# Special store rows dealt out again over the DMA engines: two more engines take three each, seven take one fewer, one takes one more

## The reference

```python
kv = einsum('bhsd,bhse->bhde', k, v)            # 8 batches, 8 heads, 576 rows, 64 columns
out = einsum('bhsd,bhde->bhse', q, kv)
x = out / rms(out) * g_norm                     # as 4608 tokens x 512
logits = x @ phi                                # 32 slots: 8 experts x 4
slot_input = softmax(logits, over tokens).T @ x
slot_out[e] = relu(slot_input[e] @ w1[e]) @ w2[e]
return softmax(logits, over slots) @ slot_out   # 4608 x 512, float32
```

## Time and profile before

| | |
|---|---|
| median of 3 runs | 171.88 us (171.63 to 171.92) |
| the profiled execution's own time | 171.93 us |
| its span, first to last instruction | 170.6 us |
| outside the span | 1.3 us |
| busy share of the span: PE, ACT, DVE, POOL | 87%, 52%, 51%, 35% |
| DMA engines, mean busy share in nearly all slices | 0.9 or more |
| moved | 71.63 MB, mean 420 GB/s |

### The profile page before, as it was taken

The page is one execution under the profiler, slowest core; times in us unless marked ns, Lnnn a source line. Parts: engine busy times, 40 slices in busy tenths (PEclk is TensorE's granted clock), DMA queues, the critical chain, the costliest instruction groups (busy, mean ns, idle before and its releaser), DMA issues.

```text
span 170.6 us, 3976 instructions
## 1 busy us (share of the span) xinstructions
PE 148.2 (87%) x1704; PEld 100.6 (59%) x1704; DVE 87.4 (51%) x187; ACT 88.8 (52%) x230; POOL 59.4 (35%) x73
## 2 busy tenths in 40 slices
PE   7989699899899899999988999899969889989200
PEld 3469578799679787887885673333326543445000
DVE  1122159583677464857266998526886036318300
ACT  3036587787956888869498870204131045218300
POOL 7000707777456476382736589000000004000000
PEclk9999999999999999999999999999999999999755
DMA  5999999999999999999999899999899999999996
GB/s 184 419 421 424 440 421 438 471 423 444 458 412 423 432 441 447 454 399 454 442 423 454 380 473 414 423 408 460 366 423 434 446 434 401 424 418 422 439 447 259
DMA packets 3843, 71.63 MB, mean 420 GB/s; under 512 B 778, under 2 KB 778, under 8 KB 913
## 3 DMA queue, kind: packets, MB, share of 16 engines
q1 hardware_dynamic: 3425, 71.20, 97.7%
q0 software_dynamic: 400, 0.18, 0.4%
HBM read 61.94 MB, written 9.44 MB: 418 GB/s over the span
## 4 chain that ended last, share of the span: by engine, by line
PE 49%; DMA 29%; ACT 11%; DVE 3%; SPq 2%; issue 1%
PE psum L93 49%; DMA arena<-in_w_dram 15%; DMA arena<-in_kv_dram 14%; ACT arena L93 3%; ACT bd L93 3%; ACT sq L93 2%; SPq L93 2%; ACT part L93 1%; DVE ms L93 1%; ACT r L93 1%; ACT d L93 1%; DVE logits L93 1%; DVE d L93 0%; DVE part L93 0%; DVE arena L93 0%
## 5 line engine op out<-in xcount | busy, mean ns | idle before, releaser
L93 PE MATMUL psum<-bd,arena 128*128 128x192 f32 (+1 forms) x320 | 54.8, 335 | 2.8 <-ACT bd L93 1.6
L93 PEld LDWEIGHTS psum<-bd,arena 128*128 128x128 f32 (+1 forms) x320 | 45.2, 179 | 8.4 <-ACT bd L93 2.8
L93 PE MATMUL psum<-arena 128*64 128x64 f32 (+2 forms) x896 | 36.3, 270 | 1.9 <-DMA arena<-in_kv_dram 1.0
L93 PEld LDWEIGHTS psum<-arena 128*64 128x64 f32 (+2 forms) x896 | 27.5, 129 | 14.6 <-issue 4.8
L93 DVE TENSOR_REDUCE ms<-sq 128x16 f32<-128x1024 f32 (+1 forms) x19 | 22.1, 1163 | 26.5 <-ACT sq L93 26.0
L93 POOL TENSOR_TENSOR arena<-arena,r 128x512 f32<-128x512 f32 x34 | 34.7, 1042 | 0.0
L93 POOL TENSOR_TENSOR part<-part,r 128x512 f32<-128x512 f32 x17 | 17.8, 1048 | 47.9 <-DVE r L93 47.9
L93 ACT COPY arena<-psum 128x512 f32<-128x512 f32 (+2 forms) x48 | 30.7, 649 | 6.0 <-PE psum L93 5.9
L93 ACT ACTIVATE sq<-psum 128x512 f32<-128x512 f32 x36 | 21.5, 597 | 9.6 <-PE psum L93 9.2
L93 ACT COPY part<-psum 128x256 f32<-128x256 f32 (+1 forms) x38 | 13.6, 359 | 12.6 <-DVE part L93 11.4
L93 DVE TENSOR_REDUCE logits<-part 128x64 f32<-128x512 f32 (+1 forms) x18 | 17.8, 991 | 0.1
(11 more groups left out here) (77 smaller groups left out, 110.0 us busy)
## 6 DMA issues: line engine op xcount, KB each, us to landing
arena<-in_w_dram SPq DMA_DIRECT2D x2, 8064.0 KB, 30.2
arena<-in_t_dram SPq DMA_DIRECT2D x1, 6912.0 KB, 37.5
arena<-in_w_dram SPq DMA_DIRECT2D x1, 6400.0 KB, 23.0
arena<-in_w_dram SPq DMA_DIRECT2D x3, 2048.0 KB, 19.2
arena<-in_kv_dram SPq DMA_DIRECT2D x2, 2304.0 KB, 23.7
arena<-in_kv_dram SPq DMA_DIRECT2D x1, 4608.0 KB, 42.8
arena<-in_w_dram SPq DMA_DIRECT2D x1, 4096.0 KB, 25.8
arena<-in_kv_dram SPq DMA_DIRECT2D x1, 3584.0 KB, 32.4
```

The source lines that it names most:

```text
L93: self.inst, self.token = method(*args, **kwargs), None
```

## The change

Special chunk-rows on each engine:

| engine | 0 | 1 to 4, each | 5, 6 | 7, 8, each | 9, 10 | 11, 12, each | 13, 14 | 15 |
|---|---|---|---|---|---|---|---|---|
| before | 11 | 6 | 0 | 10 | 0 | 0 | 0 | 9 |
| after | 10 | 5 | 0 | 9 | 0 | 3 | 0 | 10 |

In all seven chunk-rows are taken, one from each of seven engines, and seven are given: three each to engines 11 and 12, one to 15. The total stays 64. GpSimd's queue issues three stores in place of two: behind the one for 7 and 8 a step of two (over 9 and 10), the store for 11 and 12, another step of two (over 13 and 14), and the store for 15, which now has 5 partitions of both chunks. A step no longer waits for the one before it and reads and writes rows of its own; SP waits for every step at the end. No bytes are added except those of the steps.

```diff
 FIRST = (
-    ("sync", 1, 4, 30, 5, 1, 0, 1), ("sync", 121, 4, 2, 3, 3, 0, 1), ("sync", 117, 4, 3, 2, 2, 1, 2),
-    ("gpsimd", 1, 4, 20, 2, 1, 1, 2), ("gpsimd", 81, 4, 9, 2, 2, 1, 2),
+    ("sync", 1, 4, 25, 5, 1, 0, 1), ("sync", 101, 4, 2, 3, 3, 0, 1), ("sync", 97, 4, 3, 2, 2, 1, 2),
+    ("gpsimd", 1, 4, 18, 2, 1, 1, 2), ("gpsimd", 73, 4, 6, 2, 1, 1, 2), ("gpsimd", 109, 4, 5, 2, 2, 0, 2),
     ("sync", 3, 4, 32, 1, 1, 0, 2), ("sync", 0, 2, 64, 1, 1, 0, 3), ("sync", 1, 2, 64, 1, 1, 2, 3),
 )
-STEPS = (7, 6)
+STEPS = (7, 2, 2)
...
-    stepped_over = [None]
+    stepped_over = []
 
     def step_over(n):
-        ends = [x[:n, : 2 * w].rearrange("p (c n) -> p c n", c=2)[:, :, :4] for x, w in ((stepped, 8), (first_in, 64))]
-        stepped_over[0] = dma(pool, *ends, after=[stepped_over[0]])
+        at = sum(STEPS[: len(stepped_over)])
+        rows = slice(at, at + n)
+        ends = [x[rows, : 2 * w].rearrange("p (c n) -> p c n", c=2)[:, :, :4] for x, w in ((stepped, 8), (first_in, 64))]
+        stepped_over.append(dma(pool, *ends) if n else None)
...
-    for token in [*stores[:-1], stepped_over[0]]:
+    for token in filter(None, [*stores[:-1], *stepped_over]):
         nc.sync.wait_ge(*token)
```

## The result

Over 20 runs each, the changed kernel has a median of 172.23 us against 171.80; the ratio is 1.0018, with a 95% interval of 1.0010 to 1.0025. By the medians it is slower by 0.43 us, a quarter of a per cent; the ratio, which takes all runs with their two levels, is just under a fifth of a per cent. Both are clearly more than nothing.

What follows compares the result with a forecast made beforehand. The prediction took the slowest of 16 DMA engines to bound the kernel. Its terms, 0 + 0.42 + 0 + 0.03, gave +0.45 us on the profiled 171.93, and 172.3 against the median; range 171.8 to 172.65.

Steps and rivals of the forecast that it cites:

- Term 2: Three chunk-rows more on engines 11 and 12 delay the end by +0.42 us, bounds 0 and +0.69.
- lone late start: Profile sign: one or two last packets start alone at 169.6 to 170.0, 0.3 to 0.7 us behind the rest.
- A: The forecast: engine 11 or 12 is among the nine late engines, end moves +0.2 to +0.75 us; chance 0.70.
- C: Engines 11 and 12 have one fetch each and absorb their rows; end unchanged, 171.9 us with small packets; chance 0.12.
- Term 1: One chunk-row fewer on engines 0 to 4, 7 and 8: value 0, bounds -0.23 and 0 us.
- Term 3: One chunk-row more on engine 15: bounds 0 and +0.23 us, nothing in the sum.
- rival B: 11 and 12 are early; engine 15's tenth chunk-row sets the end, +0.1 to +0.23 us; chance 0.13.
- Terms 4, 5 and 6: GpSimd's two more DMA instructions and small packets, +0.03 us; later rows holding up last store, nothing; SP's extra waits, nothing.
- term 4: GpSimd's queue issues two more DMA instructions: later issue costs nothing, added small packets 0 to +0.1 us, taken as +0.03.

Runs made afterwards that it cites:

- six rows: Six chunk-rows on each of engines 11 and 12, three fewer each on 7 and 8, against the changed kernel; 172.76 to 173.20 and two lower, ratio 1.0052.
- the last kernel above: Against the kernel before: one chunk-row fewer on each of eight fetching engines, four more each on 7 and 8, one more on 0, one fewer on 15; 172.61 us.
- 13 and 14 again: Second measurement of the changed kernel with its six chunk-rows on engines 13 and 14 instead of 11 and 12; ratio 1.0027, one run at 171.64.
- 9 and 12: The changed kernel with its six chunk-rows on engines 9 and 12, three each, measured twice; median of all 172.39 us, ratios 1.0030 and 1.0033.
- seven on 12: Seven chunk-rows on engine 12, none on 11, one fewer on engine 0, against the changed kernel; ratio 1.0048, heaps at 171.87 to 172.02 and 172.93 to 173.41.
- one row each, cut astray: One chunk-row each on 11 and 12, taken from 7 and 8, against the kernel before, the two rows one contiguous piece; 173.41 us, ratio 1.0068.
- one row each, mended: One chunk-row each on 11 and 12, taken from 7 and 8, cut so they cannot merge, against the kernel before; 171.91 us, ratio 1.0007.

## Why the prediction was right

**The bound.** That the end is the slowest of 16 DMA engines, and that only the dealing of rows matters, holds in each kernel: moves of a few packets made levels of up to 2 us, and the traces show the last engines alone.

**Term 2, three rows on 11 and 12: +0.42 with bounds 0 and 0.69.** The upper level stands 0.45 above before, and six rows raise it to a median of 173.1, 1.3 above. The step and its size were right for four executions in five. The lone late start that the prediction described, at 169.6 to 170.0, is not in the changed kernel's trace, whose last start is before 169.1; it is in that of the same load on 13 and 14, at 169.6 to 169.7.

**The strings of packets.** In the trace of before, of the 1823 packets that start after 100 us and end before 168, 1814 have another that starts 3 to 5 ns before their end, and at 13 moments from 144 to 166 us 16 packets are under way each time. So the records can be strung into 16 strings, each the work of one engine; where two continuations fit, I take the one with which every string has the even transfers of SP's queue in the same order, eight packets of each. In the trace of before one string then carries 11 special chunk-rows of SP's queue, four carry six, GpSimd's nine for engine 15 are on one, and of its 20 for 7 and 8 ten are on one string, eight and two on two others (a wrong link), as the kernel deals them. With the fetches of a trace numbered 1 to 13 in time, a fetch and the eighth after it are on one string in 58 of 65 cases, in the 13 traces that could be strung so (all but that of the last kernel above), and 6, 7 and 8 have no second one in 38 of 39. That is a turn around eight engines, five of them with two. That they are PE's fetches is inferred from counts: between one and the next PE and its weight loads start 211 to 328 instructions, while ACT, DVE and POOL start 235, 197 and 81 in the whole trace. In the trace of before the strings of 6, 7 and 8 start their last packet at 167.55, 167.75 and 168.05, those of 1 and 9, 4 and 12, 2 and 10 at 168.85, 169.08 and 169.32, and those that carry 11 and 13 at 168.88 and 168.98. In the traces with rows on engines that fetch:

| kernel, traced run | rows: fetches of their strings, last start | last start of all others |
|---|---|---|
| changed, 171.68 | three: 7, 168.09; three: 8, 168.17 | 169.06 (2 and 10) |
| 13 and 14 again, 171.64 | three: 6, 168.75; three: 7, 168.39 | 169.04 (11) |
| 13 and 14, 172.29 | three: 6, 168.29; three: 5 and 13, 169.62 | 169.11 |
| 9 and 12, 172.11 | three: 8, 168.00; three: 3 and 11, 169.51 | 168.91 |
| 9 and 12 again, 172.48 | three: 3 and 11, 169.87; three: none found, 168.17 | 169.11 |
| six rows, 173.17 | six: 3 and 11, 170.56; six: 4 and 12, 170.42 | 169.10 |
| seven on 12, 173.35 | seven: 4 and 12, 170.70 | 169.11 |
| one row each, cut astray, 172.13 | nine: 6, 169.53 | 169.02 |
| one row each, mended, 171.96 | one: 1 and 9, 169.34; one: 2 and 10, 169.29 | 169.17 |

Three rows on a string with one fetch end before the last of the others; three or more on one with two fetches, and nine on one with one, end behind all strings without such rows.

**Rivals A and C.** I set them against each other as one being true. Both are, by the levels: A in 16 of 20 executions, C in 4. The last sentence of the prediction named as a sign of its being wrong that the engines that fetch might change from one execution to the next, and they do. So the picture of one fixed turn was wrong. The median hit all the same because a median shows only the commoner level; had the lower level been the commoner one, the same mechanism would have given some 171.6. The changing turn should have been a rival with a forecast of its own, two levels. The chance of 0.11 that 11 and 12 are both single was too low by the prediction's own picture: the three single engines are neighbours in the turn, which makes it 2 in 8. I read from one trace that 6, 9, 10, 11 and 12 carried two fetches, which came from the packets strung together; strung the same way, the traced run of the changed kernel begins its turn at 13, those of the others at 6, 9, 10 or 11, always in the order of the numbers. In the lower runs whose traces there are (changed kernel, 13 and 14), the loaded pair has one fetch each. In the upper ones that could be strung, at least one has two; with seven rows on 12 the string that carries them has the fetches at 46.9 and 139.0 us and starts its last packet at 170.70, where the next to last string does so at 169.11. No view numbers the engines, and the strings have some wrong links, so this rests on counts and levels as well: low runs 7 of 44 for a neighbouring pair with three or six rows (changed kernel, 13 and 14, six rows), 0 of 11 for the pair that is never single, 9 of 23 for one engine. Equally likely beginnings would give 11, 0 and 8.6. That they are equally likely is not shown: 7 is on the low side of 11 (seven or fewer of 44 would come up with a chance of 0.11).

**Term 1, relief worth nothing, bounds -0.23 and 0.** In the median nothing: the kernel with the rows on 7 and 8 keeps the relief of 0 to 4 and is level with before. The lower level, 0.17 under before's median, may be this relief; four runs are too few to say so.

**Term 3 and rival B, engine 15.** Ten rows there cost nothing (the rows-on-7-and-8 kernel, interval up to 1.0003). By the strings, engine 15 starts its last packet at 169.23 in the trace of before, last but one of all; 7 and 8, with a row more each, do so at 168.07 and 168.28. In the changed kernel it is 168.74 against 168.13 and 168.30, with a row more on 15. The strings come from times and sizes alone, and in neither trace did 15 set the end. Why it is later than 7 and 8 in both is not shown.

**Terms 4, 5 and 6.** The added transfers of GpSimd measured -0.05, within noise of the +0.03 taken; the other two stayed at nothing, as the issue times show. In the trace of before the 371 small packets of GpSimd's queue stand on all 16 strings, 15 to 28 on each and 25 on ten of them; term 4 took 23 on each.

The forecast of 172.3 met 172.23, but the runs, 171.42 to 172.58, scatter over 1.16 us, more than the 0.85 of my range, and all four of the lower level lie below it.

**The price of a fetch.** The slack of an engine with one fetch was set too low, at 1.0 us. Six rows (1.38 us) fit into it without a trace in two runs, seven on one engine (1.61) nearly: their lower heap has a median of 171.93 against 171.88. I had counted the fetch's own packet and not the one behind it. In the trace of before the fetch that starts at 129.07 takes 5.86 x 0.16 = 0.94 us, and the 16 KB packet that starts as it ends takes 6.91 x 0.16 = 1.11 us in place of 0.61:

```profile
129.07:129.08 0.01, 0.01 (x5) 0.01 (x1) 0.01 (x1) 0.00 (x0) 0.00 (x0) 1.00 5.86 1638
129.99:130.00 0.01, 0.01 (x8) 0.01 (x4) 0.01 (x1) 0.00 (x0) 0.00 (x0) 1.00 6.91 1638
```

Together a fetch took 0.94 + 0.50 = 1.44 us here. That fits the slack, and the 1.5 us between the heaps with nine rows on one engine, both of which lie above before. That the two packets are on one engine is inferred from their times. Over the 13 traces the 166 fetches that are on strings took 0.88 to 1.08 us, 0.94 in the median, so the "at least 0.97" of the prediction was one packet's time; and in all 149 cases in which a packet of SP's queue comes next on the string, it took 0.36 to 0.57 us, 0.49 in the median, longer than the median of its size within 3 us.

## What to carry to other kernels

Where a kernel is bound by its DMA engines to the last packet, find out which of them also fetch instructions, and put nothing extra on them: here a row fewer on seven engines was worth nothing that the median shows and at most the 0.17 us of the lower level, and three rows more on an engine with two fetches cost 0.45 of their 0.69 us, six 1.3 of 1.38. Look at the spread of the runs before the median: two heaps with a gap say that the kernel's fate is decided by something that changes between executions, and one trace then shows only one of the cases. Change which engines take the load (neighbours, distant ones, one alone) and count how often each heap comes up; that identifies a cause that no view names.

## What the runs showed of the hardware

- An instruction fetch of 16 KB took 0.97 us of a DMA engine against 0.61 for a plain packet of that size, and 0.88 to 1.08 in 13 traces; the packet that starts as a fetch ends was 0.50 us longer too, 0.36 to 0.57 in 149 cases; one loaded engine made heaps 1.1 us (seven rows) and 1.5 us (nine rows) apart, by their medians 171.9 and 173.1, and 172.1 and 173.7.
- The 13 fetches of an execution went in turn around eight engines: a fetch and the eighth after it are on one string of packets in 58 of 65 cases, and in the trace of before the strings with one fetch start their last packet at 167.55 to 168.05, those with two at 168.85 to 169.32.
- Which engines do the extra fetch differs from one execution of the same program to the next, as the two levels and the strings of packets show; no view gives it directly.
- A store from GpSimd of two partitions whose destination is one contiguous piece put its two rows on two engines that SP's special rows use, and the nine rows behind it on one that fetches (last start 169.53, all others by 169.02): +1.6 us in the median, and nothing clear of noise (1.0007, 0.9998 to 1.0016) when the two partitions were cut in half.
- Two kernels with a tenth transfer on SP's queue near the first stores scattered to 172.8 and 173.5, by a cause that the traces taken do not show.
